# A branch hint and a repeated wait on VectorE in a fused attention and expert kernel on one core

## What is computed

```python
def _moe_ref(x, w_in, w_out):
    h = x @ w_in
    g = np.where(h >= 1, h, np.where(h <= -1, 0.0, (h + 1) ** 2 / 4.0))
    return (g @ w_out).astype(np.float32)

def _moe2_ref(x, w_skip, w_gate, w1, w2):
    do_compute = x @ w_skip > 0
    out = x.copy()
    if not do_compute.any():
        return out
    xc = x[do_compute]
    ...
    out[do_compute] = xc + y
    return out
```

## Time and profile before

| | us |
|---|---|
| median of 3 runs | 506.06 |
| lowest and highest run | 505.82, 506.15 |
| the profiled execution | 506.15 |
| its span | 504.3 |
| PE busy | 494.1 (98%) |
| DVE busy | 253.7 (50%) |
| ACT busy | 194.4 (39%) |
| POOL busy | 212.7 (42%) |

### The profile page before, as it was taken

How to read it: one execution, slowest core, us unless ns; L and a number is a source line. 1 busy time by engine, 2 the same in 40 slices (tenths; PEclk the granted TensorE clock), 3 DMA queues, 4 the chain that set the end, 5 groups by cost and what they waited for, 6 DMA issues and landing times.

```text
span 504.3 us, 8896 instructions
## 1 busy us (share of the span) xinstructions
PE 494.1 (98%) x3427; PEld 426.6 (85%) x3427; DVE 253.7 (50%) x595; ACT 194.4 (39%) x435; POOL 212.7 (42%) x235
## 2 busy tenths in 40 slices
PE   8899999999999999999999999999999999999996
PEld 4588888889988888888888888888998898888895
DVE  5977656633335636676534666652435242332322
ACT  4974655543223324343433343433322222322222
POOL 0669877662223224465532555652222322222221
PEclk9999999999999999999999999999999999999999
DMA  8994211103001204102110421000200018840001
GB/s 270 315 388 151 73 37 45 52 2 125 1 1 48 74 23 174 51 31 60 70 48 1 173 81 34 1 2 17 106 20 1 1 22 313 292 168 1 2 1 66
DMA packets 18977, 42.15 MB, mean 84 GB/s; under 512 B 2054, under 2 KB 3920, under 8 KB 18932
## 3 DMA queue, kind: packets, MB, share of 16 engines
q1 hardware_dynamic: 18580, 41.13, 24.0%
q10 hardware_dynamic: 256, 0.41, 0.2%
q0 software_dynamic: 96, 0.02, 0.0%
HBM read 32.94 MB, written 8.78 MB: 83 GB/s over the span
## 4 chain that ended last, share of the span: by engine, by line
PE 89%; DVE 4%; ACT 3%; DMA 1%; issue 1%; POOL 0%; SPq 0%; DVEq 0%
PE bank L1046 39%; PE bank L1030 39%; PE bank L832 4%; PE bank L869 3%; PE bank L849 2%; ACT prob_first L1557 1%; DMA qk<-in_qk_dram 1%; PE bank L973 1%; PE bank L954 1%; DVE sum_terms L1191 1%; DVE prob_first L1165 1%; DVE prob L1181 1%; ACT g_hi L1684 0%; DVE bank L1174 0%; DVE row_max L1169 0%
## 5 line engine op out<-in xcount | busy, mean ns | idle before, releaser
L1787 POOL TENSOR_TENSOR g_lo<-act_f,g_hi 128x384 fp32r<-128x384 f32 x96 | 97.5, 1016 | 196.7 <-ACT g_hi L1684 196.2
L1675 ACT ACTIVATE act_f<-act_f,half_col 128x384 f32<-128x384 f32 x96 | 59.2, 616 | 200.7 <-DVE act_f L1414 200.7
L1414 DVE TENSOR_SCALAR act_f<-bank 128x384 f32<-128x384 f32 x96 | 53.4, 556 | 146.3 <-PE bank L1030 141.4
L1030 PE MATMUL bank<-x_hi,win_hi 128*128 128x384 f32 x384 | 87.7, 347 | 0.6 <-DVE act_f L1417 0.6
L1046 PE MATMUL bank<-wout_hi,g_hi 128*128 128x512 f32 x285 | 85.0, 406 | 0.0
L1684 ACT CAST g_hi<-act_f 128x384 fp32r<-128x384 f32 x96 | 49.2, 513 | 92.1 <-DVE act_f L1417 91.8
L1030 PE MATMUL bank<-x_hi,win_lo 128*128 128x384 f32 x384 | 83.9, 337 | 0.0
L1030 PE MATMUL bank<-x_lo,win_hi 128*128 128x384 f32 x384 | 83.1, 334 | 0.0
L1046 PE MATMUL bank<-wout_lo,g_hi 128*128 128x512 f32 x285 | 81.1, 393 | 0.0
L1046 PE MATMUL bank<-wout_hi,g_lo 128*128 128x512 f32 x285 | 81.0, 392 | 0.0
L1030 PEld LDWEIGHTS bank<-x_hi,win_hi 128*128 128x128 f32 x384 | 66.7, 188 | 8.3 <-issue 1.5
(11 more groups left out here) (130 smaller groups left out, 418.1 us busy)
## 6 DMA issues: line engine op xcount, KB each, us to landing
w_early<-in_w_dram SPq DMA_DIRECT2D x4, 2048.0 KB, 8.7
qk<-in_qk_dram SPq DMA_DIRECT2D x12, 592.0 KB, 5.0
out_dram<-y_rows SPq DMA_DIRECT2D x18, 256.0 KB, 2.6
win_raw<-in_w_in_dram SPq DMA_DIRECT2D x16, 256.0 KB, 9.7
wout_raw<-in_w_out_dram SPq DMA_DIRECT2D x16, 256.0 KB, 9.2
y_dram<-y_rows SPq DMA_DIRECT2D x15, 256.0 KB, 2.9
v<-in_v_dram SPq DMA_DIRECT2D x6, 384.0 KB
v<-in_v_dram SPq DMA_DIRECT2D x6, 288.0 KB
```

What stands on the lines that cost most here:

```text
L1030: mm = pe.matmul(h_ps[s % 2][:, 0:CH], w[:, f, P * k:P * (k + 1)], x[:, k, cols], start=(at == 0), stop=(at == len(order) - 1))
L1414: dve.tensor_scalar(tile, h_ps[s % 2][:, 0:CH], -1.0, 1.0, ALU.max, ALU.min).then_inc(clip_ready, 1)
L1675: act.activation(tile, tile, ACT.Square, bias=half_col[:, 0:1], scale=0.5).then_inc(square_ready, 1)
L1787: pool.tensor_tensor(g_lo[:, s % RING, :], act_f[:, s % 2, :], g_hi[:, s % RING, :].bitcast(F32), ALU.subtract).then_inc(g_lo_ready, 1)
```

## The change

Two things are added, both on DVE. In `keep_sums` each of the two copies of chunks 1 to 4 also waits for `row_skips` to have reached 3c, the count after the three `row_skip` jobs of the chunk before. Ahead of step 88 DVE's stream gets a hint instruction, and `for_tiles` on DVE is handed its location, so that DVE's branch of line 630 is marked as likely taken, as PE's already is. Nothing else differs; PE, ACT, POOL and SP run the same instructions.

```diff
@@ keep_sums, vector engine @@
                 for t in (0, 2):
                     if c > 0:
                         dve.wait_ge(y_stored[t], 32 * c)
+                        dve.wait_ge(row_skips, CT * c)
                     dve.tensor_copy(y_rows[:, t, :], y_ps[t][:, :]).then_inc(y_dve, 1)
@@ the steps, vector engine @@
             for s in range(STEPS):
+                if s == HINT_STEP:
+                    the_end_is_likely = dve.mark_branch_hint_location()
                 c, f, tile = s // FT, s % FT, act_f[:, s % 2, :]
@@ after the steps, vector engine @@
-            for_tiles(dve, first, tile)
+            for_tiles(dve, first, tile, the_end_is_likely)
```

## The result

The changed kernel takes 509.12 us (median of 6 runs, 508.52 to 510.26), the kernel before 505.97 us (6 runs, 505.82 to 506.15). The ratio is 1.0063, with a 95% interval of 1.0052 to 1.0075: slower by 0.6%, or 3.2 us. The forecast was no change, 506.1 us, in a range that ended at 506.7. The result lies outside it, on the side to which I gave 3 in 100.

The account below looks back on a forecast made before the run. PE, busy 494.1 of 504.3 us, bounds the kernel; SP's last store sets the end. 506.15 (profiled) + 0.0 waits + 0.0 hint - 0.0 branch = 506.15, put at 506.1 us for the run spread; range 505.5 to 506.7.

Parts of the forecast that it names:

- Part one: Four added waits in DVE's `keep_sums`: always met, price only their issue, 21 ns each; 0.0 us, at most 0.08.
- Part three: DVE's branch at line 630: drain gains 0.2 us, under 0.4 us of slack before SP's drain; worth 0.0 us.
- the four signs of being wrong: SP's drain moves with DVE's; instruction packet between DVE's branch and drain; DVE's drain behind 504.1; time around span not 1.85 us.
- Part two: Hint instruction on DVE ahead of step 88: about 50 ns, hidden in DVE's 2.6 us wait; 0.0 us, up to 0.05.
- Rival 3: At DVE's branch: hint loses the next block, a 2.0 us stop, end 1.5 us later, 507.6 us; chance 0.03.
- Rivals 1 and 2: Kernel's end: DVE's lateness on the path, 505.7 us, chance 0.04; hint pays outside the span, 504.2 us, chance 0.03.

Follow-up runs that it names:

- filler kernel: The changed kernel with both new waits, but a plain DVE semaphore increment in place of the hint and no hint on DVE's branch: 510.11 us, ratio 1.006.

## Why the prediction was wrong

**What bounds the kernel, and the slack.** The reading of the tail was right: SP's store sets the end in the kernel before, and DVE had 0.4 us to spare. The sum followed it correctly as long as DVE's time behind the branch could only change by 0.4 us either way. It changed by 3.0.

**Part one, the waits: the step that failed.** I wrote that the four waits are always met and that "their price is their issue", with 0.08 us as the upper bound. Their issue is as cheap as expected. Line 1395 of the changed kernel holds eight wait instructions, the four that were there and the four new ones:

```profile
L1395 DVEq EVENT_SEMAPHORE  x8: 21/36/50, 191.6 to 429.0; - x8
```

The four new ones, ahead of the second copies, take 21 ns each, as forecast; the four that were there now wait for two semaphores and take 50 ns in place of 21, which the forecast had left out. Neither reaches PE: its wait at the end of chunk 4 is 368 ns as in the earlier trace rows, and the waits of all engines between 457 and 498 us are those of the earlier trace rows. What was missing in the sum is a second price of an instruction: its length in the stream, which moves everything behind it. Four instructions were enough (the waits alone, 509.48 us), and one was not (the hint alone, 505.87 us). Eight in code that is never run did the same to the target. The term should have read: 0, or else 3.0 us more from DVE's branch to its drain less the 0.4 us of slack, so 2.6 us, depending on where the code behind the branch lies in its block. With the 0.2 us by which this execution ran late from the start, that is the 2.8 us of the span.

**Part three, the branch.** The observation that no instruction packet moved around DVE's branch was right, and so, by the missing stop (0.6 us from branch to drain), was its conclusion that DVE waited for no fetch in the kernel before. The mistake was to carry this over to a kernel whose stream had become longer, without asking how many instructions were left to the edge. One more did no harm, and four more did. The window in which I looked for a packet, 0.6 us from branch to drain, was also short: where an engine does stop, the packets start about 1.0 us behind its branch (PE's at 503.9 us in the kernel without PE's hint, its branch at 502.9), so it is the missing stop that speaks for code that was there. Two of the four signs of being wrong came, the drain behind 504.1 us and a packet between branch and drain.

**Part two, the hint.** Right in its price, 56 ns on DVE and no effect, but for a reason that I did not see. It is read behind DVE's last fetch before the branch, and both places behind that fetch (steps 78 and 88) did nothing; at both places before it (steps 60 and 70) it removes the very stop that the waits cause. (Eight steps were left at the hint, not nine, and DVE waited in each; nothing hangs on it.)

**Rival 3** had the right place, the right sign and the right kind of event, a missing block behind the branch, and its price came out at 1.5 us where the profile shows 2.8. The nearest row, 2.0 us from issue to landing of a store, was too short: DVE's drain came 3.0 us later behind its branch than before. But its cause was wrong. I held the hint responsible, and without the hint the stop is the same (filler kernel). Its 3 in 100 were a guess about hints; the question that mattered was the place of the target, which no rival asked. Rivals 1 and 2 did not occur: DVE's branch did not become faster, and the time around the span stayed.

## What to carry to other kernels

An instruction costs its issue (21 ns for each new wait here) and its place: before a long branch at the end of a kernel, look in which block of code the target lies and how many instructions are left to its edge, because adding four cheap instructions, or lengthening code that is never run, can cost what I read as a whole fetch: 3.0 us more behind DVE's branch in the changed kernel, and 3.1 us of the time for the waits alone, 2.5 us for the eight increments. On DVE a hint against this was only good where it was read before the engine's last fetch ahead of the branch, at 399.2 us, 104 us ahead of it (good at 332.2 and 379.1 us), and not merely long before the branch (void at 411.6 us); on PE it worked at 484.3 us, behind that fetch, too. If a small change costs a few us at the very end, a filler kernel of the same length tells in one run whether it is the instructions or their number.

## What the runs showed of the hardware

The stop behind a branch, which I read as a wait for code, lasted about as long on both engines: 3550 ns on PE, where it counts as the branch's own duration, and 3.6 to 4.1 us from the start of the branch to the next instruction on DVE, where the branch's own row stays at 72 or 84 ns and the stop is invisible in it. Without the stop the same way takes 0.4 us on PE and 0.6 to 0.7 us on DVE.

The two engines treated a hint differently here. On PE a hint at 484.3 us, behind PE's last fetch in the steps (474.5 us in the kernel before), was followed by a fetch that the kernel before does not have, and it worked. On DVE neither a hint at 411.6 us, which stayed void, nor one at step 60 (332.2 us), which worked, added a packet. That the timely hint replaces the block that would be next in order is the reading that fits all runs with a hint on DVE, but it was not shown by itself: it would take a hinted branch that is not taken.

Where the edge lies exactly, between one and four more instructions, was not looked for, and what lies behind it is not settled. What follows is an estimate from the recorded instructions. It takes blocks of 128, and takes it that one is fetched when DVE enters the block ahead of it. DVE's branch is the 824th in the kernel before and the 828th or 829th in the kernels with the four waits. The packet that the kernel with 45 more instructions has at 473.0 us comes after 828 of them, and the one at 399.2 us of the changed kernel after 699, so a block ends at about the 828th instruction and the next one at about the 956th. A target 122 places behind the branch would then stand at about 946 before, 950 or 951 with the waits, and 954 with the eight increments, inside in every case. Either what is missing is an instruction some places behind the target (0.5 us pass from the end of DVE's branch to its drain before the change, with no recorded instruction), or the count is off by a few. That the four waits bring the branch itself to the edge, so that the next block is only on its way, would explain them too, but not the eight increments, which leave the branch where it was.
